# Two results of a doubling level in one PSUM bank, moved by one ScalarE copy

## The chip, the cores and the metric

One Trainium2 chip, of which the kernel uses one core. The metric is device time in microseconds (us), lower is better. The core has TensorE (PE in the rows; its weight loads are shown apart as PEld), VectorE (DVE), ScalarE (ACT), GpSimd (POOL) and SyncE (SP), each with its own in-order queue; they meet by semaphores.

## The reference

The computation has three parts: a delta-rule attention over 4 x 8 heads of 768 tokens with 48 channels, then a mixture of 8 experts with Sinkhorn routing, then a gated feed-forward. The change lies in the first:

```
k_n = k / (np.linalg.norm(k, axis=-1, keepdims=True) + 1e-06)
state = np.zeros((B, H, D, D), dtype=np.float32)
for t in range(S):
    kt, vt, bt = (k_n[:, :, t], v[:, :, t], beta[:, :, t, None])
    y[:, :, t] = np.einsum('bhd,bhde->bhe', q[:, :, t], state)
    v_old = np.einsum('bhde,bhd->bhe', state, kt)
    state = state + bt[:, :, :, None] * np.einsum('bhd,bhe->bhde', kt, vt - v_old)
...
logits = x @ w_gate      # routing, 8 Sinkhorn rounds, out += P[:, e] * (relu(x @ w1[e]) @ w2[e])
...
h = x @ w_in             # g = h * sigmoid(1.702 h), result g @ w_out
```

## The kernel before

The attention takes 4 heads at a time (8 groups) and cuts the 768 tokens into 6 chunks of 128. In a chunk the recurrence is a unit triangular system of 128 x 128 for each head. The kernel builds the inverse of that matrix by doubling: from blocks of 2 rows at level 1 to blocks of 128 after level 6. It keeps the inverse, x, and its transpose, xt, both in fp16, since TensorE wants the stationary operand transposed. A level is four steps:

1. level_y on TensorE (L298): the off-diagonal part of the matrix, a_r, times x, into a PSUM bank (the first product of a level);
2. level on VectorE (L569): that result times a mask, into yp in SBUF;
3. level_x (L309) and level_xt (L317) on TensorE: xt with yp gives the new blocks of x, yp with xt the new blocks of xt. L309 is the second product and L317 the transpose product. Level 6 has no level_x;
4. on ScalarE a copy of each into x (L460) and xt (L465), fp32 in the bank, fp16 in SBUF.

Two chunks, a pair, go through the levels together, as stream 0 and stream 1. Each step of a stream is four matmuls of 128x64, one for each head, so a row "x8" is the step of both streams. Each stream has two banks (2 + 2a + n % 2, b_lev at L175), in which level n's results alternate; of a bank only the first half, 256 fp32 words, is used.

There are 24 pairs (8 groups of 3). The program is written as one body for each pair, in which each engine does three things at three distances: the serial chain (ser) of pair p, the levels (dbl) of pair p + 1 and the preparation (pre) of pair p + 2. The order of the instructions in a body is written out by hand, on each engine by itself (TensorE L409 to L440, ScalarE L500 to L513, VectorE L640 to L661); nothing is reordered afterwards. Fifteen bodies out of the middle are five rounds of a loop on the device, the rest are written out. The chain of a chunk, on TensorE, is key_state (L332), solve (L344), product with lp (L355), correct (L365), outputs (L377 to L386). Ahead of product, correct and outputs stand 10, 10 and 4 filler matmuls on the identity (L324). grams (L279) and first_x (L287) belong to the preparation. In a body the first chunk's chain lies beside levels 1 to 3, and the second's beside levels 4 to 6.

Waits that matter here: the next level's L298 waits for the x copy of its stream (act_x), L309 for yp and for the level before's xt copy (act_xt), L355 for the copy of z0 (L469) on ScalarE, L365 for VectorE's residual (L594).

After the attention the dense part runs (L863 on), on TensorE nearly without gaps.

## Time and profile before

| | |
|---|---|
| median of 3 runs | 2610.67 us (2607.55 to 2611.66) |
| span of the profiled execution | 2601.5 us |
| between that span and the median of the runs | 9.2 us |
| TensorE matmul / weight load busy | 2491.3 us (96%) / 2238.2 us (86%) |
| VectorE, ScalarE, GpSimd busy | 1054.2 us (41%), 584.0 us (22%), 648.5 us (25%) |
| TensorE idle before L309, of it for VectorE's yp | 20.6 us, 11.4 us |
| TensorE idle before L298 (all at the loop's returns) | 11.6 us |

The profiled execution gives its span; its own time is not listed apart from those of the runs, so the span and the 9.2 us to the median are what a sum is made against. Matmuls overlap one another, so the start of a row to the start of the next says how long a group held the queue; the row's own length includes what the last matmul took to drain. A slice of the page is 65 us; the attention is the first eight. The granted clock (PEclk) is a share of 2.4 GHz.

### The profile page before, as it was taken

How to read it: one execution, taken by the hardware profiler on the slowest of the kernel's cores; microseconds unless marked ns; L12 is line 12 of the kernel's file. 1: busy time of each engine (PE TensorE's matmuls, PEld its weight loads, DVE VectorE, ACT ScalarE, POOL GpSimd, SP SyncE). 2: the span in 40 equal slices, each digit the busy share in tenths (PEclk: the TensorE clock that was granted, in tenths of full speed). 3: DMA queues.
4: the chain of work that ended last, by engine and by line, in shares of the span. 5: the costliest groups of instructions: out<-in, count | busy, mean ns of one | idle time of the engine just before them, and what ended most of it. 6: DMA issues, size and time to landing. Idle time of an engine off the chain costs nothing.

```text
span 2601.5 us, 42564 instructions
## 1 busy us (share of the span) xinstructions
PE 2491.3 (96%) x17329; PEld 2238.2 (86%) x17329; DVE 1054.2 (41%) x2147; ACT 584.0 (22%) x1326; POOL 648.5 (25%) x545
## 2 busy tenths in 40 slices
PE   6988889869999999999999999999999999999999
PEld 5877778738998998998998998998999999999998
DVE  5877778554333333333333333333333333223222
ACT  4444444321111111111111111111111112222222
POOL 5555555240100101101101001001001001444532
PEclk9999989979999999999999999999999999999999
DMA  2111111010000000000000000000000000000001
GB/s 76 49 45 45 45 45 55 22 43 7 25 1 24 25 1 26 13 12 25 13 13 25 13 13 25 13 13 25 13 13 25 1 25 1 25 13 13 13 13 61
DMA packets 54612, 61.72 MB, mean 24 GB/s; under 512 B 2336, under 2 KB 46624, under 8 KB 54432
## 3 DMA queue, kind: packets, MB, share of 16 engines
q1 hardware_dynamic: 54432, 58.97, 7.3%
q8 instruction: 156, 2.56, 0.4%
q14 instruction: 24, 0.20, 0.0%
HBM read 54.24 MB, written 4.72 MB: 23 GB/s over the span
## 4 chain that ended last, share of the span: by engine, by line
PE 78%; DVE 2%; issue 0%; ACT 0%
PE bank L955 38%; PE bank L928 38%; PE bank L874 1%; PE bank L907 0%; DVE x_hl L1085 0%; DVE rowsum L1165 0%; PE bank L973 0%; DVE route L1169 0%; DVE route L1181 0%; PE bank L863 0%; DVE gated L1080 0%; DVE h_hl L1103 0%; DVE gate_hl L1071 0%; ACT x_hl L994 0%; PE bank L882 0%
## 5 line engine op out<-in xcount | busy, mean ns | idle before, releaser
L928 PE MATMUL bank<-x_hl,w_hl 128*128 128x512 f32 x4320 | 1022.8, 394 | 2.9 <-issue 2.9
L955 PE MATMUL bank<-w_hl,h_hl 128*128 128x384 f32 x5760 | 1019.5, 335 | 0.0
L955 PEld LDWEIGHTS bank<-w_hl,h_hl 128*128 128x128 f32 x5760 | 1003.4, 188 | 10.0
L928 PEld LDWEIGHTS bank<-x_hl,w_hl 128*128 128x128 f32 x4320 | 811.5, 188 | 178.3 <-issue 4.5
L1014 ACT ACTIVATE h_hl<-bank 128x512 fp32r<-128x512 f32 x384 | 229.7, 598 | 1379.7 <-PE bank L928 1379.7
L1103 DVE SCALAR_TENSOR_TENSOR h_hl<-bank,h_hl 128x512 fp32r<-128x512 f32 x384 | 265.7, 692 | 584.7 <-ACT h_hl L1014 584.5
L808 POOL TENSOR_TENSOR w_hl<-w_raw,ones 128x1536 fp32r<-128x1536 f32 x40 | 109.9, 2748 | 1378.9 <-PE bank L928 1054.7
L1127 DVE SCALAR_TENSOR_TENSOR x_tok<-bank,route,x_tok 128x384 f32<-128x384 f32 x384 | 237.3, 618 | 499.2 <-PE bank L955 499.2
L849 POOL TENSOR_TENSOR h_hl<-gated,h_hl 128x512 fp32r<-128x512 f32 x96 | 123.4, 1291 | 318.8 <-ACT h_hl L1024 318.8
L814 POOL TENSOR_TENSOR w_hl<-w_raw,w_hl 128x1536 fp32r<-128x1536 f32 x40 | 140.7, 3518 | 2.7
L1116 DVE TENSOR_TENSOR gated<-bank,sig 128x512 f32<-128x512 f32 x96 | 66.4, 692 | 166.0 <-ACT sig L1033 117.6
L460 ACT CAST x<-bank 128x256 f16<-128x256 f32 x240 | 81.2, 375 | 182.3 <-PE bank L309 181.4
L1033 ACT ACTIVATE sig<-bank 128x512 f32<-128x512 f32 x96 | 57.4, 598 | 281.7 <-PE bank L928 281.7
L569 DVE TENSOR_TENSOR yp<-bank,mask 128x256 f16<-128x256 f32 x288 | 108.4, 418 | 26.2 <-PE bank L298 26.1
L709 POOL TENSOR_TENSOR a_r<-lp,mask 128x256 f16<-128x256 f32 x96 | 70.0, 729 | 175.9 <-DVE lp L558 175.9
L465 ACT CAST xt<-bank 128x256 f16<-128x256 f32 x288 | 94.8, 388 | 35.2 <-PE bank L317 33.2
L324 PE MATMUL bank<-ident 128*128 128x128 f16 x1152 | 92.6, 226 | 0.0
L558 DVE SCALAR_TENSOR_TENSOR lp<-bank,bg,mask 128x256 f32<-128x256 f32 x192 | 83.1, 476 | 11.7 <-PE bank L279 11.0
L309 PEld LDWEIGHTS bank<-yp,xt 128*128 128x128 f16 x960 | 46.7, 104 | 44.9 <-issue 27.0
L309 PE MATMUL bank<-yp,xt 128*128 128x64 f16 x960 | 58.0, 196 | 20.6 <-DVE yp L569 11.4
L298 PE MATMUL bank<-x,a_r 128*128 128x64 f16 x1152 | 64.1, 197 | 11.6 <-issue 10.6
L1139 DVE TENSOR_TENSOR x_tok<-x_tok,bank 128x384 f32<-128x384 f32 x72 | 39.9, 554 | 85.9 <-PE bank L955 85.9
(99 smaller groups left out, 1512.5 us busy)
## 6 DMA issues: line engine op xcount, KB each, us to landing
w_raw<-in_moe_w SPq DMA_DIRECT2D x32, 768.0 KB, 4.4
kq_t<-in_kq_rows SPq DMA_DIRECT2D x48, 256.0 KB, 3.3
kv<-in_kv_cols SPq DMA_DIRECT2D x24, 384.0 KB, 3.7
out<-x_tok SPq DMA_DIRECT2D x6, 768.0 KB, 3.5
w_raw<-in_moe_w_in SPq DMA_DIRECT2D x4, 768.0 KB, 4.3
w_raw<-in_moe_w_out SPq DMA_DIRECT2D x4, 768.0 KB, 4.5
mask<-in_masks SPq DMA_DIRECT2D x1, 576.0 KB, 4.6
beta_t<-in_beta_cols SPq DMA_DIRECT2D x1, 96.0 KB, 2.9
```

What stands on the lines that cost most here:

```text
L309: m = pe.matmul(b_lev(a, lev, lev)[:, u, :, :], xt[:, c, u, :], blocks(yp[:, a, lev - 1, :, :], lev, 0)[:, u, :, :], start=True, stop=True)
L324: pe.matmul(bank[:, b, 3 * P:4 * P], ident16[:, :], ident16[:, :], start=True, stop=True)
L465: act.copy(blocks(xt[:, c, :, :], lev, 1), b_lev(a, lev + 1, lev)).then_inc(act_xt[a], 1)
L569: dve.tensor_tensor(blocks(yp[:, a, lev - 1, :, :], lev, 0), b_lev(a, lev + 1, lev), keep.to_broadcast([P, GH, P >> (lev + 1), 1 << lev]), ...
L808: pool.tensor_tensor(dst[:, 0, :, :], raw[:, :, :], ones[:, 0:1].unsqueeze(2).to_broadcast([P, k, f]), ALU.mult).then_inc(pool_whi, 1)
L814: pool.tensor_tensor(dst[:, 1, :, :], raw[:, :, :], dst[:, 0, :, :].bitcast(F32), ALU.subtract).then_inc(pool_w, 1)
L849: pool.tensor_tensor(h_hl[:, s % 2, 1, f, :], gated[:, n % 2, :], h_hl[:, s % 2, 0, f, :].bitcast(F32), ALU.subtract).then_inc(pool_lo, 1)
L928: m = pe.matmul(bank[:, f, :], w1_hl[par][:, a, kc, f * P:(f + 1) * P], x_hl[:, c, kc, b * TB:(b + 1) * TB], start=n + kc == 0, stop=n == ...
L955: m = pe.matmul(bank[:, 4 + t, 0:DM], h_hl[:, b % 2, a, f, t * P:(t + 1) * P], w2_hl[par][:, c, f, :], start=n + f == 0, stop=n == len(PAR ...
L1014: act.activation(h_hl[:, b % 2, 0, f, :], bank[:, f, :], ACT.Relu).then_inc(act_h, 1)
L1103: dve.scalar_tensor_tensor(out=h_hl[:, b % 2, 1, f, :], in0=bank[:, f, :], scalar=0.0, in1=h_hl[:, b % 2, 0, f, :].bitcast(F32), op0=ALU.m ...
L1127: dve.scalar_tensor_tensor(out=dst, in0=bank[:, 4 + t, 0:DM], scalar=route[:, b * TT + t, col], in1=dst, op0=ALU.mult, op1=ALU.add).then_i ...
```

## The change

x and xt become the two planes of one buffer xx, for each chunk plane 0 for x and plane 1 for xt. The new x blocks of a level lie in plane 0 at even positions and the new xt blocks in plane 1 at odd ones, so one access pattern with a step between planes (grown) reaches both. In PSUM each stream now has one bank instead of two: its first half takes level_y's result and then, once VectorE has read that, level_x's; its second half takes level_xt's. ScalarE moves both halves with one copy on levels 1 to 5; level 6 has xt alone, as before. The four semaphore pairs pe_x, act_x, pe_xt, act_xt become two, pe_xx_lev (raised behind level_xt) and act_xx_lev (raised by the copy). level_y of a level waits for act_xx_lev, on level 1 also for the last copy of the pair before, since the bank is now the same. level_x waits for VectorE alone. Banks 4 and 5 are no longer used by the levels.

```diff
@@ -117,10 +117,8 @@
             sem, ("pe_g", "dve_lp", "pool_at", "pool_xt", "pe_x1", "act_x1"))
         pe_y = [sem(f"pe_y_stream{a}") for a in range(2)]
         dve_y = [sem(f"dve_y_stream{a}") for a in range(2)]
-        pe_x = [sem(f"pe_x_stream{a}") for a in range(2)]
-        act_x = [sem(f"act_x_stream{a}") for a in range(2)]
-        pe_xt = [sem(f"pe_xt_stream{a}") for a in range(2)]
-        act_xt = [sem(f"act_xt_stream{a}") for a in range(2)]
+        pe_xx_lev = [sem(f"pe_xx_lev_stream{a}") for a in range(2)]
+        act_xx_lev = [sem(f"act_xx_lev_stream{a}") for a in range(2)]
         pe_ks, dve_r, dve_rl, pe_z0, act_z0 = map(sem, ("pe_ks", "dve_r", "dve_rl", "pe_z0", "act_z0"))
         pe_az, dve_res, dve_resl, pe_xr, dve_z = map(sem, ("pe_az", "dve_res", "dve_resl", "pe_xr", "dve_z"))
         pe_kz, pe_out, dve_state, act_yo = map(sem, ("pe_kz", "pe_out", "dve_state", "act_yo"))
@@ -156,8 +154,8 @@
 
             lp = sb("lp", [P, NCH, GH, 2 * P], ctx=at)
             a_r = sb("a_r", [P, NCH, GH, P], F16, ctx=at)
-            xt = sb("xt", [P, NCH, GH, P], F16, ctx=at)
-            x = sb("x", [P, NCH, GH, P], F16, ctx=at)
+            xx = sb("xx", [P, NCH, 2, GH, P], F16, ctx=at)
+            x, xt = xx[:, :, 0, :, :], xx[:, :, 1, :, :]
 
 
             yp = sb("yp", [P, 2, NLEV - 1, GH, P], F16, ctx=at)
@@ -172,10 +170,21 @@
 
             BT, BS, BO = 0, 6, 7
 
-            def b_lev(a, n, lev):
-
-                return bank[:, 2 + 2 * a + n % 2, 0:GH * P // 2].rearrange(
+            def b_lev(a, w, lev):
+
+                return bank[:, 2 + a, w * GH * P // 2:(w + 1) * GH * P // 2].rearrange(
                     "p (u m r) -> p u m r", u=GH, r=1 << lev)
+
+            def grown(c, lev):
+
+                r = 1 << lev
+                first = xx[:, c, 0, 0, 0:1]
+                return bass.AP(first.tensor, first.offset,
+                               [first.ap[0], [GH * P + r, 2], [2 * r, GH * P // (2 * r)], [1, r]])
+
+            def b_grown(a, lev):
+
+                return bank[:, 2 + a, :].rearrange("p (w m r) -> p w m r", w=2, r=1 << lev)
 
             def blocks(t, lev, odd):
 
@@ -291,32 +300,31 @@
                         a = c % 2
                         if lev == 1:
                             pe.wait_ge(act_x1, j + 1)
+                            wait(pe, act_xx_lev[a], (NLEV - 1) * p)
                         else:
 
-                            pe.wait_ge(act_x[a], (NLEV - 2) * p + lev - 1)
+                            pe.wait_ge(act_xx_lev[a], (NLEV - 1) * p + lev - 1)
                         for u in range(GH):
-                            m = pe.matmul(b_lev(a, lev + 1, lev)[:, u, :, :], a_r[:, c, u, :],
+                            m = pe.matmul(b_lev(a, 0, lev)[:, u, :, :], a_r[:, c, u, :],
                                           blocks(x[:, c, :, :], lev, 0)[:, u, :, :], start=True, stop=True)
                         m.then_inc(pe_y[a], 1)
 
                     def level_x(g, c, j, p, lev):
                         a = c % 2
 
-                        wait(pe, act_xt[a], (NLEV - 1) * p + lev - 1)
                         pe.wait_ge(dve_y[a], (NLEV - 1) * p + lev)
                         if lev < NLEV - 1:
                             for u in range(GH):
-                                m = pe.matmul(b_lev(a, lev, lev)[:, u, :, :], xt[:, c, u, :],
-                                              blocks(yp[:, a, lev - 1, :, :], lev, 0)[:, u, :, :],
-                                              start=True, stop=True)
-                            m.then_inc(pe_x[a], 1)
+                                pe.matmul(b_lev(a, 0, lev)[:, u, :, :], xt[:, c, u, :],
+                                          blocks(yp[:, a, lev - 1, :, :], lev, 0)[:, u, :, :],
+                                          start=True, stop=True)
 
                     def level_xt(g, c, j, p, lev):
                         a = c % 2
                         for u in range(GH):
-                            m = pe.matmul(b_lev(a, lev + 1, lev)[:, u, :, :], yp[:, a, lev - 1, u, :],
+                            m = pe.matmul(b_lev(a, 1, lev)[:, u, :, :], yp[:, a, lev - 1, u, :],
                                           blocks(xt[:, c, :, :], lev, 1)[:, u, :, :], start=True, stop=True)
-                        m.then_inc(pe_xt[a], 1)
+                        m.then_inc(pe_xx_lev[a], 1)
 
                     def keep_busy(b, n):
 
@@ -338,7 +346,7 @@
 
                         wait(pe, act_yo, j)
                         pe.wait_ge(dve_rl, j + 1)
-                        pe.wait_ge(act_xt[c % 2], (NLEV - 1) * (p + 1))
+                        pe.wait_ge(act_xx_lev[c % 2], (NLEV - 1) * (p + 1))
                         for u in range(GH):
                             for n in range(2):
                                 m = pe.matmul(b_ser(BO)[:, u, :], xt[:, c, u, :], rhs_hl[:, n, u, :],
@@ -454,15 +462,13 @@
                         act.wait_ge(pe_x1, j + 1)
                         act.copy(x[:, c, :, :], b_x1()).then_inc(act_x1, 1)
 
-                    def level_x(g, c, p, lev):
+                    def level(g, c, p, lev):
                         a = c % 2
-                        act.wait_ge(pe_x[a], (NLEV - 2) * p + lev)
-                        act.copy(blocks(x[:, c, :, :], lev, 0), b_lev(a, lev, lev)).then_inc(act_x[a], 1)
-
-                    def level_xt(g, c, p, lev):
-                        a = c % 2
-                        act.wait_ge(pe_xt[a], (NLEV - 1) * p + lev)
-                        act.copy(blocks(xt[:, c, :, :], lev, 1), b_lev(a, lev + 1, lev)).then_inc(act_xt[a], 1)
+                        act.wait_ge(pe_xx_lev[a], (NLEV - 1) * p + lev)
+                        if lev < NLEV - 1:
+                            act.copy(grown(c, lev), b_grown(a, lev)).then_inc(act_xx_lev[a], 1)
+                        else:
+                            act.copy(blocks(xt[:, c, :, :], lev, 1), b_lev(a, 1, lev)).then_inc(act_xx_lev[a], 1)
 
                     def solved(g, c, j):
                         act.wait_ge(pe_z0, j + 1)
@@ -481,11 +487,8 @@
                         def levels(lev):
                             if dbl is not None:
                                 g, c, p = dbl
-                                if lev < NLEV - 1:
-                                    level_x(g, c, p, lev)
-                                    level_x(g, c + 1, p, lev)
-                                level_xt(g, c, p, lev)
-                                level_xt(g, c + 1, p, lev)
+                                level(g, c, p, lev)
+                                level(g, c + 1, p, lev)
 
                         def prep(a, what):
                             if pre is not None:
@@ -566,7 +569,7 @@
                         a = c % 2
                         dve.wait_ge(pe_y[a], (NLEV - 1) * p + lev)
                         keep = blocks(mask[:, LEVEL + lev:LEVEL + lev + 1, :], lev, 0)
-                        dve.tensor_tensor(blocks(yp[:, a, lev - 1, :, :], lev, 0), b_lev(a, lev + 1, lev),
+                        dve.tensor_tensor(blocks(yp[:, a, lev - 1, :, :], lev, 0), b_lev(a, 0, lev),
                                           keep.to_broadcast([P, GH, P >> (lev + 1), 1 << lev]),
                                           ALU.mult).then_inc(dve_y[a], 1)
 
```

On ScalarE the levels of a body change as follows, levels 4 and 5 of one body, with the second chunk's z0 copy and the roots of a later pair between them. Before (xt and x are the two buffers, pe_x and pe_xt TensorE's two products):

```order
L460 CAST x<-bank 128x16x16 [waits pe_x_stream0]
L460 CAST x<-bank 128x16x16 [waits pe_x_stream1]
L465 CAST xt<-bank 128x16x16 [waits pe_xt_stream0]
L465 CAST xt<-bank 128x16x16 [waits pe_xt_stream1]
L469 COPY z<-bank 128x192 [waits pe_z0]
L451 ACTIVATE root<-ss 128x8 [waits dve_ss]
L460 CAST x<-bank 128x8x32 [waits pe_x_stream0]
L460 CAST x<-bank 128x8x32 [waits pe_x_stream1]
L465 CAST xt<-bank 128x8x32 [waits pe_xt_stream0]
L465 CAST xt<-bank 128x8x32 [waits pe_xt_stream1]
```

and after, at the same place (xx is the shared buffer):

```order
L469 CAST xx<-bank 128x2x16x16 [waits pe_xx_lev_stream0]
L469 CAST xx<-bank 128x2x16x16 [waits pe_xx_lev_stream1]
L475 COPY z<-bank 128x192 [waits pe_z0]
L459 ACTIVATE root<-ss 128x8 [waits dve_ss]
L469 CAST xx<-bank 128x2x8x32 [waits pe_xx_lev_stream0]
L469 CAST xx<-bank 128x2x8x32 [waits pe_xx_lev_stream1]
```

Four copies of 256 columns have become two of twice 256, and the wait is on the later of the two products. No other instruction of ScalarE changes its place.

TensorE's matmuls keep their order; what they wait for changes. Before, from level 4's first product to level 5's (grams, then level 4's second and transpose products, then solve):

```order
L298 MATMUL bank<-x,a_r 128x64 [waits act_x_stream0]
L298 MATMUL bank<-x,a_r 128x64 x3
L298 MATMUL bank<-x,a_r 128x64 [waits act_x_stream1]
L298 MATMUL bank<-x,a_r 128x64 x3
L279 MATMUL bank<-kq_t 128x256 [waits act_x1,ld_kq5]
L279 MATMUL bank<-kq_t 128x256 x3
L309 MATMUL bank<-yp,xt 128x64 [waits dve_y_stream0,act_xt_stream0]
L309 MATMUL bank<-yp,xt 128x64 x3
L309 MATMUL bank<-yp,xt 128x64 [waits dve_y_stream1,act_xt_stream1]
L309 MATMUL bank<-yp,xt 128x64 x3
L317 MATMUL bank<-xt,yp 128x64 x8
```

and after, at the same place:

```order
L308 MATMUL bank<-xx,a_r 128x64 [waits act_xx_lev_stream0]
L308 MATMUL bank<-xx,a_r 128x64 x3
L308 MATMUL bank<-xx,a_r 128x64 [waits act_xx_lev_stream1]
L308 MATMUL bank<-xx,a_r 128x64 x3
L288 MATMUL bank<-kq_t 128x256 [waits act_x1,ld_kq5]
L288 MATMUL bank<-kq_t 128x256 x3
L318 MATMUL bank<-yp,xx 128x64 [waits dve_y_stream0]
L318 MATMUL bank<-yp,xx 128x64 x3
L318 MATMUL bank<-yp,xx 128x64 [waits dve_y_stream1]
L318 MATMUL bank<-yp,xx 128x64 x3
L325 MATMUL bank<-xx,yp 128x64 x8
```

The first product's wait has moved from the x copy to the copy of both, and the second product's wait for ScalarE is gone.

## Rows read from the trace of the kernel before

**Rows 1.** page, busy tenths in 40 slices, and the chain that ended last by engine.

```profile
PE   6988889869999999999999999999999999999999
...
PE 78%; DVE 2%; issue 0%; ACT 0%
```

**Rows 2.** busy time by stretches: PE, PEld, DVE, ACT, POOL (x instructions), PEclk, DMA share, GB/s.

```profile
98.80:108.60 9.80, 8.06 (x146) 7.41 (x146) 7.96 (x23) 4.61 (x15) 5.34 (x8) 1.00 0.23 70
276.10:285.90 9.80, 5.51 (x91) 4.67 (x90) 6.59 (x19) 2.66 (x8) 4.90 (x8) 0.95 0.23 70
285.90:295.80 9.90, 9.38 (x108) 9.38 (x108) 4.14 (x12) 3.21 (x10) 4.80 (x6) 0.53 0.01 3
305.60:315.50 9.90, 8.90 (x147) 7.96 (x147) 8.44 (x26) 4.18 (x13) 5.43 (x9) 1.00 0.21 68
```

**Rows 3.** timeline, levels 3 and 4: start us, us, engine, line, what, [idle before].

```profile
316.30 0.40 PE L317 MATMUL bank<-xt,yp 128*128 128x64 f16 x8
...
316.53 0.40 PE L298 MATMUL bank<-x,a_r 128*128 128x64 f16 x8
...
316.85 0.73 PEld L279 LDWEIGHTS bank<-kq_t 64*128 64x128 f32 x8
316.86 1.13 PE L279 MATMUL bank<-kq_t 64*128 64x256 f32 x8
...
317.50 0.75 DVE L569 TENSOR_TENSOR yp<-bank,mask 128x256 f16<-128x256 f32 x2
...
317.97 0.70 PE L309 MATMUL bank<-yp,xt 128*128 128x64 f16 x8
...
318.50 0.40 PE L317 MATMUL bank<-xt,yp 128*128 128x64 f16 x8
...
318.74 0.36 PE L344 MATMUL bank<-rhs_hl,xt 128*128 128x48 bf16 x8
...
318.94 0.48 PE L298 MATMUL bank<-x,a_r 128*128 128x64 f16 x8
...
319.26 0.72 PE L324 MATMUL bank<-ident 128*128 128x128 f16 x10
319.50 0.35 ACT L469 COPY z<-bank 128x192 f32<-128x192 f32 x1
...
319.98 0.97 PEld L355 LDWEIGHTS bank<-z,lp 128*128 128x128 f32 x8 [0.17 <-POOL a_r L709]
```

**Rows 4.** timeline, level 5.

```profile
320.90 0.40 PE L309 MATMUL bank<-yp,xt 128*128 128x64 f16 x8
...
321.14 0.40 PE L317 MATMUL bank<-xt,yp 128*128 128x64 f16 x8
321.22 0.65 ACT L460 CAST x<-bank 128x256 f16<-128x256 f32 x2 [1.27 <-PE bank L309]
...
322.63 0.37 PE L365 MATMUL bank<-res_hl,xt 128*128 128x48 bf16 x8 [0.54 <-DVE res_hl L594]
...
322.84 0.39 PE L298 MATMUL bank<-x,a_r 128*128 128x64 f16 x8
```

**Rows 5.** timeline, level 6 and level 1 of the next pair.

```profile
325.29 0.40 PE L317 MATMUL bank<-xt,yp 128*128 128x64 f16 x8
...
326.03 0.40 PE L298 MATMUL bank<-x,a_r 128*128 128x64 f16 x8
...
327.82 0.70 PE L309 MATMUL bank<-yp,xt 128*128 128x64 f16 x8 [0.33 <-DVE yp L569]
```

**Rows 6.** groups by line, whole run: busy us, mean ns | idle before.

```profile
L569 DVE TENSOR_TENSOR yp<-bank,mask 128x256 f16<-128x256 f32 x288 | 108.4, 418 | 26.2 <-PE bank L298 26.1
L465 ACT CAST xt<-bank 128x256 f16<-128x256 f32 x288 | 94.8, 388 | 35.2 <-PE bank L317 33.2
...
L460 ACT CAST x<-bank 128x256 f16<-128x256 f32 x240 | 81.2, 375 | 182.3 <-PE bank L309 181.4
...
L455 ACT COPY x<-bank 128x512 f16<-128x512 f16 x48 | 28.1, 585 | 55.4 <-PE bank L287 55.4
```

## The prediction

> **What bounds the kernel now.** I read the page first, for where the end is set. The chain that ended last is TensorE for 78% of the span, and it lies in the dense part, where TensorE is at nine tenths or more in every slice [rows 1]. The change touches nothing there. It touches the attention part, the first eight of the forty slices, which ends at about 520 us. The dense part waits for all of it, so what attention gains or loses moves the end one for one. In attention TensorE is at eight to nine tenths, its in-order queue being the longest of the five. The second view is the busy time by stretches: in an ordinary stretch of 9.9 us TensorE is busy for 8.90, VectorE for 8.44 and ScalarE for 4.18 [rows 2]. ScalarE, whose work the change cuts, has more than half its time free. So fewer ScalarE instructions are worth something only where TensorE waits for one. The third view, the timeline, shows how little it waits now.
>
> Call S the start of the transpose product of a level (L317). The rows give, for level 3, S = 316.30: the next level's first product (L298) starts at S + 0.23, the grams (L279) at S + 0.56, level 4's second product (L309) at S + 1.67 and its transpose product at S + 2.20 [rows 3]. For level 4, S = 318.50: solve (L344) at S + 0.24, L298 at S + 0.44, the ten filler products (L324) at S + 0.76, and the product with lp (L355) at S + 1.48, after a wait of 0.17 [rows 3]. For level 5, S = 321.14: the correction (L365) at S + 1.49, L298 at S + 1.70 [rows 4]. For level 6, S = 325.29: L298 at S + 0.74, and L309 a full 2.53 us behind S [rows 5]. Levels 1 and 2 of the next pair repeat levels 4 and 5, since the serial chain stands in the same places.
>
> **What goes away.** As the order of ScalarE's instructions shows, each level from 1 to 5 has four ScalarE copies of 128x256 now, and two of 128x512 after. The whole run has 240 x copies of 375 ns and 288 xt copies of 388 ns [rows 6]; 240 of each become 240 larger ones, 48 stay. That relieves an engine with time to spare. Also gone is level_x's wait for the xt copy of the level before, and the trace has next to nothing waiting there: L309 waits for VectorE. I put both at nothing.
>
> **What is added.** Now x is copied while TensorE still runs the transpose product, and the next L298 follows that copy alone. After the change one copy needs both products, so it cannot start before the transpose product has written, and L298 needs its end. A wait appears on TensorE's in-order queue, with everything of the serial chain and of the next pair queued behind it.
>
> How long it is: a copy starts 0.32 us after the product that feeds its stream has begun (L309 at 320.90, copy at 321.22 [rows 4]). The trace has no fp32-to-fp16 copy of 128x512, so its price is bounded. From below: no more than a 128x256 one, 0.375. From above: two such copies behind one another, 0.65 us for the pair [rows 4]. The nearest row is the ScalarE copy of 128x512 fp16 out of a bank, 585 ns [rows 6], and I take 0.59. For the second stream, two 256 copies take 0.65 together, so the second starts 0.27 behind the first; the larger one adds 0.59 - 0.38 = 0.21, giving 0.48. Stream 0 is then copied at S + 0.91 and stream 1 at S + 1.39. With about 0.06 for the signal (estimate: L309 at 317.97 starts 0.05 after the first of the VectorE pair at 317.50 [rows 3] has run its 0.418 [rows 6]), L298 runs its first half at S + 0.97, its second at S + 1.45, and TensorE is free of it at about S + 1.56.
>
> The Trainium skill bears on the same size. "ScalarE: Activation LUTs", section on what ACT_TABLE_LOAD costs, gives 186 ns plus 0.833 ns an element for an activation with immediates, and an overlap of about 93 ns between neighbours. By it the copy would be 613 ns, the pitch 520, and the second end 0.06 us later than mine, which over the 72 places below is 4 us more. The two rows lie a little under that rule (375 against 399 for 256, 585 against 613 for 512), so the rows are used.
>
> Level by level:
> - Levels 4 and 1: L298 used to be done at S + 0.76. Now S + 1.56, then the ten fillers (0.55 in the queue), and L355 at S + 2.11 where it was S + 1.48. The ScalarE copy of z0 ends near S + 1.39 + 0.35 = S + 1.74, before that, so the old wait of 0.17 is swallowed. Cost 0.63 each, 1.26 a pair.
> - Level 3: L298's second half at S + 1.45, grams 0.22 behind it at S + 1.67 and over at S + 2.41 (their weight loads take 0.73 [rows 3], and I round up to the 0.74). VectorE has both yp by then: it is free at 317.50, S + 1.20, starts the second 0.32 after that half's product, at S + 1.77, and ends it at S + 2.19. Level 4's L309 starts at S + 2.41, but it no longer stalls between its halves, so its transpose product starts 0.23 behind (as on level 5 [rows 4]) at S + 2.64, where it was S + 2.20. Cost 0.44 a pair.
> - Levels 5 and 2: the copies end at S + 1.39, the correction starts at S + 1.49 anyway for VectorE's sake, L298 at S + 1.70. Cover: the serial chain's own wait, with 0.25 to spare. Nothing.
> - Level 6 into level 1 of the next pair: one copy per stream as before, but L298 now writes into the same bank and so waits for it: second half near S + 0.32 + 0.65 + 0.06 = S + 1.03 against S + 0.85. L309 stands 2.53 us behind S for VectorE's sake, and that hides 0.18. Without key_state ahead of it (one body in three) L298 slips by up to 0.54, and L309 waits there too. Nothing.
>
> Sum: 1.26 + 0.44 = 1.70 us a pair. 240 x copies are 24 pairs of 5 levels and 2 streams, so 24 pairs: 41 us. The profiled execution has a span of 2601.5; with 41 it is 2642. The median of the runs is 2610.67, 9.2 above the span, and that part doesn't move: 2652.
>
> The ends. With copies at their lower bound (0.375, pitch 0.27) the second ends at S + 0.97: levels 4 and 1 cost 0.21 each, level 3 nothing, in all 0.42 x 24 = 10 us: 2621. With 0.65 for a copy and as much for the pitch, the second ends at S + 1.62, everything 0.23 later than in my sum: 1.70 + 3 x 0.23 = 2.4, 57 us: 2668.
>
> **Rivals.**
> Rival A, the clock falls. TensorE's granted clock is 1.00, which is 2.4 GHz, in nearly all stretches, and goes towards 0.5 (1.2 GHz) after the stall at the loop's return, where TensorE was busy for 5.51 of 9.8 us [rows 2]. The change adds two idle pieces at three places a pair. In the low stretch 108 matmuls run in 9.9 us against 147 at full clock [rows 2], so 9.9 us there lose 2.6. If the clock were low for half of the 510 us of attention, that is 26 stretches by 2.6, 67 us on top: 2719. Against it: by my sum a stretch of 9.9 becomes about 10.75 with the same 8.90 busy, 83%, and the row at 98.80 has 8.06 of 9.80, 82%, at clock 1.00; no new gap is near the 2.6 us that stand ahead of the fall. Chance 11%.
> The Trainium skill argues for this rival: "TensorE: Matmul & The Clock Gate", section on a second failure mode, tells of a kernel that cycled through PSUM banks and idled briefly between groups of matmuls often enough for the clock to swing. By that rule the time would be rival A's; the row at 98.80 is against it at this size of gap.
>
> Rival B, cover that I don't see. If the copies cost what their lower bound says and the fillers behind L298 absorb the rest of the wait, nothing is left: 2611, up to the 2621 above. For it: the fillers are there only to keep TensorE running, and the product behind them waited 0.17. Against it: they are instructions in the queue and run however late they are. Chance 8%.
>
> Rival C, faster: ScalarE is drained sooner. z0's copy is queued behind the level's copies, and L355 waits 0.17 for it. If two large copies end before the four small ones did (319.50 is when z0's copy starts, S + 1.00), L355 starts earlier, by 0.17 at most, in 48 places: 8 us, 2603. It decides only if the second merged copy ends before S + 1.00, so copy and pitch together under 0.68, and if L298's added wait is then also under the 0.17. Two copies of twice the size at 585 ns don't do that. Chance 4%.
>
> **Chances.** Forecast 77%, A 11%, B 8%, C 4%. The forecast's own range is 2621 to 2668; I stretch it upwards to take in the nearer half of the clock's cases and a pitch larger than assumed: 2625 to 2685. A measurement here can tell about 0.2%, 5 us. Slower by more than that: the forecast and A, 88%. Within: most of B, 7%. Faster: C and a little more, 5%.
>
> **What the profile after would show.** ScalarE copies of 128x512 fp16 from fp32, 240 of them, near 590 ns; TensorE waiting for ScalarE ahead of both halves of the next first product after levels 1, 3 and 4, in all some 1 us each time, and not after 2 and 5; L355's wait gone; ScalarE busy for less, attention ending near 560 us; the granted clock as before outside the loop's returns. It is wrong if the copies are much off 590, if level 3 costs as much as level 4 (then VectorE's stall was no cover), if levels 2 and 5 wait too, or if low clock shows in stretches where it was 1.00.

## The result and the profile after

The changed kernel takes 2639.91 us (median of 4 runs, 2630.43 to 2644.35) against 2611.07 before (4 runs, 2607.55 to 2611.66): ratio 1.0119, interval 1.0101 to 1.0136. It is slower by about 29 us (31 by the ratio); the forecast was 2652, 41 slower.

The loss is in attention. The dense part's first instruction starts at 546.91 us in the profile after and at 520.26 before, 26.7 of the 27.1 by which the spans differ (2628.6 and 2601.5). The page shows the same chain behind it [rows 1]:

```profile
PE   6888888877999999999999999999999999999999
...
PE 77%; DVE 2%; issue 0%; ACT 0%
```

The added wait is there and so is the copy's size. Groups by line of the changed kernel (line numbers are its own: L469 is the merged copy, L308 the first product, L597 the low part of the residual, which is the fp32 residual less its bf16 rounding):

```profile
L469 ACT CAST xx<-bank 128x512 f16<-128x512 f32 x240 | 128.8, 589 | 249.1 <-PE bank L325 249.1
...
L308 PE MATMUL bank<-xx,a_r 128*128 128x64 f16 x1152 | 80.0, 196 | 59.9 <-ACT xx L469 45.1 <-issue 11.4 <-ACT xx L471 1.8
...
L597 DVE TENSOR_TENSOR res_hl<-res,res_hl 128x192 bf16<-128x192 f32 x48 | 17.2, 357 | 1.6
```

240 merged copies at 589 ns stand for 480 at 375 to 388 [rows 6]. L308 now idles TensorE for 45.1 us behind L469, where its namesake L298 had no wait for ScalarE worth a row. The waits of TensorE for it in 50 to 540 us, in total, times, longest:

```profile
PE bank L308 <- ACT xx L469: 41.8, 135, 0.6
```

Levels 3 and 4 in the timeline, to be laid beside [rows 3]. S is 331.54:

```profile
331.54 0.40 PE L325 MATMUL bank<-xx,yp 128*128 128x64 f16 x8
...
331.85 1.07 ACT L469 CAST xx<-bank 128x512 f16<-128x512 f32 x2 [2.26 <-PE bank L325]
...
332.49 0.29 PE L308 MATMUL bank<-xx,a_r 128*128 128x64 f16 x4 [0.56 <-ACT xx L469]
...
332.82 0.91 DVE L572 TENSOR_TENSOR yp<-bank,mask 128x256 f16<-128x256 f32 x2
...
332.98 0.29 PE L308 MATMUL bank<-xx,a_r 128*128 128x64 f16 x4 [0.20 <-ACT xx L469]
...
333.20 1.14 PE L288 MATMUL bank<-kq_t 64*128 64x256 f32 x8
334.26 0.29 PEld L318 LDWEIGHTS bank<-yp,xx 128*128 128x128 f16 x8 [0.33 <-issue]
334.27 0.41 PE L318 MATMUL bank<-yp,xx 128*128 128x64 f16 x8
...
334.51 0.40 PE L325 MATMUL bank<-xx,yp 128*128 128x64 f16 x8
```

The first product runs in two halves at S + 0.95 and S + 1.44, each behind its half of the copy, which took 1.07 for the pair. grams follows at S + 1.66. VectorE has both yp by 332.82 + 0.91 = S + 2.19. The second product starts at S + 2.73, after 0.33 in which no engine is named. Then level 4, S = 334.51:

```profile
334.83 1.07 ACT L469 CAST xx<-bank 128x512 f16<-128x512 f32 x2 [1.68 <-PE bank L325]
...
335.47 0.29 PE L308 MATMUL bank<-xx,a_r 128*128 128x64 f16 x4 [0.36 <-ACT xx L469]
...
335.96 0.29 PE L308 MATMUL bank<-xx,a_r 128*128 128x64 f16 x4 [0.20 <-ACT xx L469]
...
336.59 0.97 PEld L363 LDWEIGHTS bank<-z,lp 128*128 128x128 f32 x8
...
337.52 0.40 PE L318 MATMUL bank<-yp,xx 128*128 128x64 f16 x8
...
337.76 0.40 PE L325 MATMUL bank<-xx,yp 128*128 128x64 f16 x8
```

The weight loads of L363 (the product with lp) start at S + 2.08 and without the old wait. Last the residual of level 5, S = 337.76:

```profile
337.57 0.73 POOL L712 TENSOR_TENSOR a_r<-lp,mask 128x256 f16<-128x256 f32 x1 [0.56 <-DVE lp L561]
...
337.73 0.35 DVE L594 TENSOR_TENSOR res_hl<-rhs,bank 128x192 bf16<-128x192 f32 x1 [0.23 <-PE bank L363]
...
338.38 0.36 DVE L597 TENSOR_TENSOR res_hl<-res,res_hl 128x192 bf16<-128x192 f32 x1
338.39 0.88 POOL L715 TENSOR_TENSOR xx<-a_r,mask 128x256 f16<-128x256 f16 x1
...
338.79 0.37 PE L373 MATMUL bank<-res_hl,xx 128*128 128x48 bf16 x8
```

The correction (L373) starts at S + 1.03. Before it was S + 1.49 [rows 4]. The low part of the residual takes 0.36, and GpSimd's L715, which starts at the same moment, takes 0.88 instead of its usual 0.67. In the kernel before the pair looked the other way round. Its timeline at the same place:

```profile
320.87 0.73 POOL L709 TENSOR_TENSOR a_r<-lp,mask 128x256 f16<-128x256 f32 x1 [0.20 <-DVE lp L558]
...
321.11 0.36 DVE L591 TENSOR_TENSOR res_hl<-rhs,bank 128x192 bf16<-128x192 f32 x1 [0.31 <-PE bank L355]
...
321.69 0.67 POOL L712 TENSOR_TENSOR xt<-a_r,mask 128x256 f16<-128x256 f16 x1
...
321.76 0.81 DVE L594 TENSOR_TENSOR res_hl<-res,res_hl 128x192 bf16<-128x192 f32 x1
...
322.63 0.37 PE L365 MATMUL bank<-res_hl,xt 128*128 128x48 bf16 x8 [0.54 <-DVE res_hl L594]
```

GpSimd starts 0.07 earlier there, and VectorE's instruction takes 0.81. In the changed kernel all 48 low parts take 357 to 359 ns. In the kernel before 34 of the 48 take 478 to 878 (median of the 48: 812), and 14 take 357 or 358. The 14 lie in bodies at the two ends of attention: in four no GpSimd instruction runs beside them, in one it is all but over, and in nine it starts between 3 ns ahead of VectorE's and 17 behind, and takes 0.87 to 0.89 itself. So the kernel before has both outcomes in one run, and some nanoseconds decide: 6 ahead were enough for GpSimd. In the changed kernel its start lies between 4 ahead and 11 behind.

What moved the two starts can be read from the rows, from level 4's transpose product (318.50 before, 334.51 after). GpSimd's a_r (L709 before, L712 after), which waits for VectorE's lp and stands right ahead of GpSimd's xt, went from S + 2.37 to S + 3.06, by 0.69. VectorE's residual (L591 before, L594 after), which follows the product with lp, went from S + 2.61 to S + 3.22, by 0.61. GpSimd lost 0.08 against VectorE, and it had been 0.07 ahead.

From one transpose product to the next, medians over the bodies at full clock, from the starts in the timelines (us):

| from level to level | 3 to 4 | 4 to 5, 1 to 2 (each) | 5 to 6 | 6 to 1 | 2 to 3 | a pair |
|---|---|---|---|---|---|---|
| before | 2.21 | 2.63 | 4.16 | 3.07 | 4.89 | 19.59 |
| changed | 2.98 | 3.25 | 3.80 | 3.07 | 4.53 | 20.88 |
| forecast of the difference | +0.44 | +0.63 | 0 | 0 | 0 | +1.70 |
| measured | +0.77 | +0.62 | -0.36 | 0.00 | -0.36 | +1.29 |

One body in three is 0.45 shorter from 5 to 6 and from 2 to 3, in both kernels, so the differences hold for it too. 1.29 by 24 pairs is 31 us. Some of it comes back at the loop's returns: the first correction of the run is 2.7 us late, the 36th 16.9 and the 48th 26.6, but at two of the returns the lag falls, from 16.9 to 15.1 and from 17.4 to 14.1. In these two profiled executions the low clock after a return is shorter in the changed kernel. Busy time by stretches, with one that holds a return and an ordinary one [rows 2]:

```profile
167.80:177.60 9.80, 6.76 (x92) 5.57 (x92) 5.24 (x16) 1.97 (x6) 2.77 (x6) 0.83 0.24 71
...
305.60:315.50 9.90, 8.51 (x145) 7.40 (x144) 6.98 (x20) 4.36 (x10) 4.41 (x7) 1.00 0.10 28
```

Behind the four returns together the clock is at its low level for 14 us, where it was for 38 before. At 2.6 us lost in 9.9 [rows 2] the 24 us of difference are worth some 6, an estimate. Over the spans the mean clock is 0.986 after and 0.982 before.

### The profile page after: what moved, and what is told of

The parts are those of the page before. It is cut to its first block, busy times and chain, and to the rows that moved or that the text cites. A ratio compares the mean times of both kernels' runs of the same rounds, so it can differ in the third digit from the quotient of the medians.

```text
span 2628.6 us, 42033 instructions
## 1 busy us (share of the span) xinstructions
PE 2503.0 (95%) x17329; PEld 2236.6 (85%) x17329; DVE 1051.0 (40%) x2147; ACT 563.2 (21%) x1086; POOL 651.9 (25%) x545
## 4 chain that ended last, share of the span: by engine, by line
PE 77%; DVE 2%; issue 0%; ACT 0%
PE bank L958 38%; PE bank L931 38%; PE bank L877 1%; PE bank L910 0%; DVE x_hl L1088 0%; PE bank L976 0%; DVE route L1172 0%; DVE route L1184 0%; PE bank L866 0%; DVE gated L1083 0%; DVE h_hl L1106 0%; DVE gate_hl L1074 0%; ACT x_hl L997 0%; DVE rowsum L1168 0%; PE bank L885 0%
## 5 line engine op out<-in xcount | busy, mean ns | idle before, releaser
L469 ACT CAST xx<-bank 128x512 f16<-128x512 f32 x240 | 128.8, 589 | 249.1 <-PE bank L325 249.1
L308 PE MATMUL bank<-xx,a_r 128*128 128x64 f16 x1152 | 80.0, 196 | 59.9 <-ACT xx L469 45.1
L572 DVE TENSOR_TENSOR yp<-bank,mask 128x256 f16<-128x256 f32 x288 | 115.3, 420 | 42.3 <-PE bank L308 37.5
L308 PEld LDWEIGHTS bank<-xx,a_r 128*128 128x128 f16 x1152 | 51.2, 98 | 82.2 <-ACT xx L469 62.5
L712 POOL TENSOR_TENSOR a_r<-lp,mask 128x256 f16<-128x256 f32 x96 | 69.8, 727 | 204.0 <-DVE lp L561 204.0
L715 POOL TENSOR_TENSOR xx<-a_r,mask 128x256 f16<-128x256 f16 x96 | 74.0, 771 | 7.5
L288 PE MATMUL bank<-kq_t 64*128 64x256 f32 x384 | 62.9, 452 | 9.4 <-DMA kq_t<-in_kq_rows 8.5
```

The costliest lines, as they stand in the source:

```text
L308: m = pe.matmul(b_lev(a, 0, lev)[:, u, :, :], a_r[:, c, u, :], blocks(x[:, c, :, :], lev, 0)[:, u, :, :], start=True, stop=True)
L469: act.copy(grown(c, lev), b_grown(a, lev)).then_inc(act_xx_lev[a], 1)
L572: dve.tensor_tensor(blocks(yp[:, a, lev - 1, :, :], lev, 0), b_lev(a, 0, lev), keep.to_broadcast([P, GH, P >> (lev + 1), 1 << lev]), ALU.m ...
```

## The experiments

A ratio is to the kernel before on the same chip. Steps from level to level are medians as in the table above.

**e1_split: the shared buffer, the copies apart.** The changed kernel with xt's result in a bank of its own, two copies a stream, and the first product waiting for the x copy alone.

```diff
-                return bank[:, 2 + a, w * GH * P // 2:(w + 1) * GH * P // 2].rearrange(
+                return bank[:, 2 + a + 2 * w, 0:GH * P // 2].rearrange(
...
-                            pe.wait_ge(act_xx_lev[a], (NLEV - 1) * p + lev - 1)
+                            pe.wait_ge(act_x[a], (NLEV - 2) * p + lev - 1)
...
-                            act.copy(grown(c, lev), b_grown(a, lev)).then_inc(act_xx_lev[a], 1)
+                        act.copy(blocks(x[:, c, :, :], lev, 0), b_lev(a, 0, lev)).then_inc(act_x[a], 1)
+                        act.copy(blocks(xt[:, c, :, :], lev, 1), b_lev(a, 1, lev)).then_inc(act_xt[a], 1)
```

> The changed kernel with the shared buffer xx kept, level_y and level_x of a stream still in one bank, but level_xt's result in a bank of its own and two copies on ScalarE again, so that the next level's first product waits for the x copy alone. Theory (the wait for the merged copy is the whole cost, less what an accident of the VectorE and GpSimd timing gives back): everything returns, 2611 within 4 us, the low part of the residual back at 0.81 us. Rival (the layout of the shared buffer, or one bank for the first and second product, costs something of itself): stays above 2616.

2610.88 us, ratio 1.0004 (0.9995 to 1.0013). Every row of the table above is back to before, within 0.01, and the low part has a median of 807 ns again. The buffer's layout and the one bank for first and second product cost nothing.

**e2_wait_only: the wait alone, nothing merged.**

```diff
                             pe.wait_ge(act_x[a], (NLEV - 2) * p + lev - 1)
+                            pe.wait_ge(act_xt[a], (NLEV - 1) * p + lev - 1)
```

> The kernel before with one line more: the next level's first product also waits for the xt copy of its stream. Four small copies, four banks, no merging. Theory: the wait is what costs, and the merged copy's size comes on top of it. With small copies the second stream's xt copy ends near S + 1.13 (level 4) in place of S + 1.39, so levels 1 and 4 cost about 0.37 each and level 3 about 0.4; if the residual's low part stays at 0.81 that is 1.1 us a pair, 2638; if it falls to 0.36 on levels 2 and 5 it is some 0.4 a pair, 2620. Rival (a wait on small copies is free since they run beside the transpose product, and all the cost is the copy's size): 2611.

2637.33 us, ratio 1.0108 (1.0093 to 1.0123). Level 3 to 4 takes 2.62 (+0.41), 4 to 5 3.21 (+0.58) and 1 to 2 3.06 (+0.42, expected +0.37 for each), and 5 to 6 and 2 to 3 are 0.36 shorter, the low part at 358 ns in 44 of 48. 6 to 1 takes 3.16 (+0.09). That is +0.79 a pair, 19 us, and the run lost 26 to 29. The rest isn't the wait for ScalarE. TensorE's waits show it under "issue":

```profile
PE bank L299 <- ACT xt L466: 30.2, 66, 0.6
PE bank L299 <- issue: 25.7, 8, 3.9
```

25.7 us in 8 pauses, against 11.4 in 4 in the changed kernel. All eight lie at the loop's four returns: one ahead of the first L299 of a body, as in every kernel here, and one of 3.3 to 3.9 us behind that single matmul, ahead of the other seven. What makes the second is open; it belongs to e2 alone, and the steps above don't contain it. The rival, a free wait, is out: the wait on small copies costs three fifths of what the merged copy costs (+0.79 against +1.29 a pair). The other 0.50 comes with the merged copy, which is larger and starts only behind the transpose product, 0.35 of it at level 3.

**e3_before_res: one SBUF input fewer.** The kernel before with the fp32 residual in PSUM.

```diff
-                        dve.tensor_tensor(res[:, :, :], rhs[:, :, :], b_ser(BS), ALU.subtract)
+                        dve.tensor_tensor(b_res(), rhs[:, :, :], b_ser(BS), ALU.subtract)
...
-                        dve.tensor_tensor(res_hl[:, 1, :, :], res[:, :, :], res_hl[:, 0, :, :], ALU.subtract
+                        dve.tensor_tensor(res_hl[:, 1, :, :], b_res(), res_hl[:, 0, :, :], ALU.subtract
```

b_res() is columns 192 to 383 of bank BS, which no matmul writes between the product and the correction.

> The kernel before with the fp32 residual written into unused columns of its own PSUM bank instead of SBUF, so that the VectorE instruction that forms the low part has one SBUF input instead of two. Theory (that instruction at 0.81 us was waiting for a GpSimd instruction that began 0.07 us before it; in the changed kernel it began just ahead and took 0.36): it takes about 0.36 in all 48 chunks, the correction starts up to 0.46 earlier, and the kernel ends 16 to 22 us earlier, 2589 to 2595. Rival (the 0.81 is that instruction's own time on this path, and in the changed kernel it is shorter since ScalarE is less busy): unchanged, 2611.

2590.34 us, ratio 0.9929 (0.9916 to 0.9943), inside the forecast and faster than both kernels. Its timeline at level 5:

```profile
322.34 0.67 POOL L714 TENSOR_TENSOR xt<-a_r,mask 128x256 f16<-128x256 f16 x1
...
322.41 0.36 DVE L596 TENSOR_TENSOR res_hl<-bank,res_hl 128x192 bf16<-128x192 f32 x1
...
322.83 0.37 PE L367 MATMUL bank<-res_hl,xt 128*128 128x48 bf16 x8
```

GpSimd again starts 0.07 ahead, as before, and VectorE takes 0.36 all the same, since only one of its inputs is in SBUF. In the run all 48 lie between 356 and 358 ns. Levels 5 to 6 and 2 to 3 are down to 3.71 and 4.44, by 0.45 each.

**e4_after_res: the same edit to the changed kernel.**

> The changed kernel with the same edit to the residual. Theory (in the changed kernel VectorE already wins the race for the read port, in the profiled run in all 48 chunks, so there is nothing left to gain): 2640, within 5 us; the spread of its runs (2630 to 2644) would shrink if they come from races lost now and then. Rival (ScalarE's load set the 0.36): 2640 as well, but then the kernel before with this edit stays at 2611. Second rival (a PSUM write costs VectorE more than an SBUF write): slower than 2645.

2639.15 us, ratio 1.0106 (1.0083 to 1.0129), runs from 2627.1 to 2644.07. No gain, as expected, since the race was already won. The spread did not shrink, so lost races don't make it. The profiled runs point at the clock: 2642.47 us at a mean of 0.978 here, 2630.43 at 0.986 in the changed kernel, with the steps of the levels alike but for 6 to 1, which is 0.2 shorter here. With the clock at 0.5 where it is low, that is 116 us of low clock against 74 (twice the missing share of the span); at 2.6 us lost in 9.9 [rows 2] the 42 us are worth 11 of the 12 between the runs. That is an estimate and not varied by an edit.

e3 and e4 also give the price of the change with the race out of both kernels: 2590.34 against 2639.15, 49 us. By levels it is +0.77 (3 to 4), +0.61 each (4 to 5, 1 to 2), +0.08 and +0.09 (5 to 6, 2 to 3) and -0.08 (6 to 1), 2.08 a pair. So levels 5 and 2 do pay a little. Once the correction starts at S + 1.03, the second half of the next first product waits for the copy: it follows the first half by 0.20 there in the changed kernel, and by 0.11 in the kernel before and e3.

**e5_nudge and e9_nudge_wide: GpSimd starts later.** The kernel before, with a memset of an unused tile on GpSimd between a_r and xt of a chunk's second half; 64 columns in e5, 384 in e9.

```diff
+                        if m == 1:
+                            pool.memset(spare[:, :], 0.0)
                         pool.wait_ge(pool_at, 3 * j + m + 1)
```

> The kernel before with nothing changed on VectorE, TensorE or ScalarE; GpSimd alone gets a small extra instruction (a memset of 64 columns of an unused tile) between a_r and xt of the second half of a chunk, so that its xt instruction begins some 0.1 us or more later. Theory (an exclusive claim on the SBUF read port, won by whoever starts first): VectorE's low part of the residual now starts first, takes 0.36 in place of 0.81, GpSimd waits instead, and the kernel is faster although it does more: 2588 to 2597. Rival (the low part is slow for another reason): 2611 or more, the low part at 0.81.

2606.97 us, ratio 0.9988 (0.9979 to 0.9997): the forecast missed, and the low part stayed at 819 ns. The edit did not do what it was to do:

```profile
333.61 0.15 POOL L713 MEMSET spare<- 128x64 f32 x1
333.75 0.67 POOL L715 TENSOR_TENSOR xt<-a_r,mask 128x256 f16<-128x256 f16 x1
...
333.81 0.83 DVE L595 TENSOR_TENSOR res_hl<-res,res_hl 128x192 bf16<-128x192 f32 x1
```

The memset filled the pause that stood behind a_r anyway, and xt still starts 0.06 ahead of the low part. So this run tells nothing between the theories, and the wider one followed.

> As e5_nudge, whose 64-column memset lay in the pause between two GpSimd instructions and moved the start of xt by nothing against VectorE's low part (323.88 against 323.95); now the memset has 384 columns and should last some 0.4 us, so that xt begins 0.1 to 0.4 us behind the low part. Theory (the read port goes to whoever starts first): the low part at 0.36 in nearly all 48 chunks, levels 2 and 5 shorter by 0.36 each, the kernel 16 to 20 us faster than before although GpSimd does more, 2589 to 2597. Rival (the port is not it): the low part stays at 0.81 and the time at 2610.

2593.97 us, ratio 0.9956 (0.9941 to 0.9970), inside the forecast, low part at 357 or 358 ns in 43 of 48:

```profile
337.82 0.42 POOL L713 MEMSET spare<- 128x384 f32 x1
...
338.04 0.36 DVE L595 TENSOR_TENSOR res_hl<-res,res_hl 128x192 bf16<-128x192 f32 x1
338.20 0.73 POOL L715 TENSOR_TENSOR xt<-a_r,mask 128x256 f16<-128x256 f16 x1
```

Now xt starts 0.16 behind the low part. 5 to 6 takes 3.80 and 2 to 3 takes 4.52, as in the changed kernel. GpSimd does more, and the kernel is 14 us faster. So the order of two starts is worth that much, with the instructions of VectorE, ScalarE and TensorE untouched.

**e10_after_dnudge: VectorE starts later, in the changed kernel.**

```diff
+                        dve.memset(spare[:, 0:16], 0.0)
                         dve.wait_ge(dve_res, j + 1)
```

> The changed kernel with the opposite nudge: VectorE gets a memset of 16 columns of an unused tile between the fp32 residual and its low part, so that the low part begins after GpSimd's xt instruction and not with it. Theory: the low part falls back to about 0.8 us, levels 2 and 5 are some 0.36 to 0.5 longer, and the change costs what my sum said and more: 48 x 0.4 = 19 us above the changed kernel, 2655 to 2665. Rival (the 0.36 of the changed kernel comes from a less busy ScalarE or the free banks): only the memset's own tenth of a microsecond, about 2644.

2634.07 us, ratio 1.0122 (1.0100 to 1.0145): missed. As in e5 the 0.07 us memset fitted into a pause (the low part ahead of or level with GpSimd's instruction, 327.66 and 327.67, and at 357 ns in all 48). So this run doesn't show the changed kernel with the race lost; e7 below does, by a third route.

**e6_after_grams: grams into the gap.** The changed kernel with two lines swapped.

```diff
-                        levels(4, level_y)
                         prep(1, grams)
+                        levels(4, level_y)
```

> The changed kernel with grams put ahead of level 4's first product on TensorE, into the wait for the merged copy. What is tested is the third of a microsecond between the end of grams and the matmuls behind them, which my sum lacked. Theory (it belongs to grams: the next weight load waits until their last matmul has drained): the gap of about 0.33 moves with grams and now stands ahead of level 4's first product, whose first half starts near S + 1.29; from level 3's transpose product to level 4's some 2.35 in place of 2.97; 15 us faster than the changed kernel, about 2625. Rival (it belongs to the second product, a signal from VectorE that comes late): first product at S + 0.97 still, no gap behind grams, the second product as late after its yp as before; about 2630.

2628.24 us, ratio 1.0069 (1.0055 to 1.0083). Level 3 to 4 takes 2.66 (2.98 in the changed kernel, 2.35 expected). The first product after grams:

```profile
332.61 1.13 PE L288 MATMUL bank<-kq_t 64*128 64x256 f32 x8
...
333.67 0.29 PEld L308 LDWEIGHTS bank<-xx,a_r 128*128 128x128 f16 x8 [0.33 <-issue]
```

L308 follows grams by 1.06, the same distance at which the second product followed grams in the changed kernel (333.20 to 334.27), and this time the idle piece stands ahead of L308. So it belongs to grams and was hidden before by L309's wait for VectorE. Whether the drain of the last matmul makes it is not shown. Level 3 to 4 stays above the expected 2.35 since the first product comes at S + 1.39, not 1.29, and the second product, which then waits for VectorE's yp again, at S + 2.20.

**e7_after_fill: the filler into the gap as well.** As e6, and the ten filler matmuls of the product ahead of the next first product.

```diff
                         chain(0, solve, True)
+                        chain(0, fill)
                         levels(2, level_y)
...
                         chain(1, solve, True)
+                        chain(1, fill)
                         levels(5, level_y)
```

> As the run before, and in addition the ten filler matmuls of the product stand ahead of the first product of levels 2 and 5 instead of behind it, so that they run in the wait for the merged copy. Theory (the whole cost of the change is TensorE standing still at three places a pair while its filler work waits behind): levels 1 and 4 fall from 3.25 to about 2.7 us (2.63 in the kernel before), in all about 2600 if the residual's low part stays at 0.36, and 2618 if its race is lost again. Rival (the merged copy costs by itself, through ScalarE or the shared bank): stays above 2620 with the low part at 0.36.

2614.80 us, ratio 1.0024 (1.0015 to 1.0033). 25 of the 29 us are back, 15 short of the forecast. Levels 1 and 4 take 2.90, not 2.7. The forecast's 2600 assumed the low part at 0.36; it is at 0.46 (L600, median 462 ns). The timeline from level 4's transpose product (334.99), with level 5's at 337.89:

```profile
334.99 0.40 PE L325 MATMUL bank<-xx,yp 128*128 128x64 f16 x8
...
335.43 0.72 PE L332 MATMUL bank<-ident 128*128 128x128 f16 x10
...
335.98 0.28 PE L308 MATMUL bank<-xx,a_r 128*128 128x64 f16 x4
...
336.43 0.29 PE L308 MATMUL bank<-xx,a_r 128*128 128x64 f16 x4 [0.17 <-ACT xx L472]
...
336.73 1.09 PE L364 MATMUL bank<-z,lp 128*128 128x48 f32 x8
337.10 0.87 DVE L564 SCALAR_TENSOR_TENSOR lp<-bank,bg,mask 128x256 f32<-128x256 f32 x2
...
337.89 0.40 PE L325 MATMUL bank<-xx,yp 128*128 128x64 f16 x8
338.05 0.73 POOL L715 TENSOR_TENSOR a_r<-lp,mask 128x256 f16<-128x256 f32 x1 [0.83 <-DVE lp L564]
...
338.53 0.46 DVE L600 TENSOR_TENSOR res_hl<-res,res_hl 128x192 bf16<-128x192 f32 x1
338.86 0.67 POOL L718 TENSOR_TENSOR xx<-a_r,mask 128x256 f16<-128x256 f16 x1
...
339.05 0.37 PE L374 MATMUL bank<-res_hl,xx 128*128 128x48 bf16 x8 [0.20 <-DVE res_hl L600]
...
339.58 0.40 PE L296 MATMUL bank<-ident,xx 128*128 128x128 f16 x4
```

The fillers hide the wait of the first half, but the second half still runs at S + 1.44 and the product with lp can only stand behind it, at S + 1.74. At level 5 something else is late. GpSimd's a_r, which follows VectorE's lp pair, starts at S + 0.16, against S - 0.19 in the changed kernel (337.57). It now begins 0.48 ahead of the low part, which takes 0.46, so the correction comes 1.16 behind the transpose product and not 1.03. GpSimd's xt ends at 338.86 + 0.67, and first_x (L296), which reads it, starts 0.05 behind that. 5 to 6 takes 3.93. e8 tells which of the two sets it.

**e8_after_fill_res: both.**

> The run before with the fp32 residual in PSUM, so that no race decides. Theory: level for level like the kernel before with the residual in PSUM (2590), plus 0.1 to 0.2 us a pair for what the gaps don't cover: 2590 to 2600. Rival (a merged copy is worth something once its wait is covered, ScalarE being drained sooner): below 2588.

2613.75 us, ratio 1.0021 (1.0010 to 1.0032): missed by 14 us, and not told apart from e7. The low part is at 357 ns and the correction at S + 1.06, but 5 to 6 stays at 3.93. So first_x behind GpSimd's xt sets that step, and not the correction: in the median it starts 0.06 behind the end of xt, in e7 and in e8. GpSimd is late because the lp pair is, and that pair stands behind a yp that waits for the second half of the copy.

e8 is 23 us slower than e3, which has four small copies. The rival, a gain from a shorter ScalarE queue, is not seen; but the wait is not covered in full here either (0.17 ahead of each second half, with the product with lp behind it), so e8 doesn't exclude a small one. In e3 there is little left to gain between 50 and 515 us: TensorE's weight loads wait 4.4 us in all, 26 times up to 0.2, ahead of the product with lp, where the z0 copy can be the cause, and 1.4 us once ahead of solve.

## Why the prediction was right, and where its terms were off

The mechanism of the wait stood: x's copy used to run beside the transpose product, the merged one cannot, and the three places without cover pay. e1 takes the wait away and the loss is gone; e2 adds only the wait and most of the loss is there.

- The copy. Forecast 0.59 and a second end at S + 1.39; measured 589 ns and, in level 4, 334.83 + 1.07 = S + 1.39.
- Levels 4 and 1, 0.63 each: measured 0.62.
- Level 3, 0.44: measured 0.77. The term mis-sized is grams, which I ended at S + 2.41 by its weight loads. The step from grams to anything behind it has 0.33 more. In the kernel before, VectorE's wait lay over it, so no row named it there. e6 moved it with grams. The prediction gave "level 3 costs as much as level 4" as a sign of being wrong, and it came true (0.77 against 0.62), though not for the reason it named: VectorE had its yp at S + 2.19, as forecast.
- Levels 5 and 2, "nothing", since "the correction starts at S + 1.49 anyway for VectorE's sake": measured -0.36 each, 17 us over 24 pairs. This is the step that failed. I took VectorE's wait for a fixed length of work. It held 0.45 of waiting for GpSimd, decided by 0.07 us, and the change's own delay of the lp instructions, behind which GpSimd is queued, shifted GpSimd by 0.08 more than VectorE. e3 and e9 show the 0.45 and how it goes away; that the shift came about in this way in the changed kernel is worked out from its timeline, and no edit varied it alone (in e7, which shifts GpSimd too, the low part is long again). The -0.36 is -0.45 for this and +0.09 for the copy (e3 and e4), whose cover of 0.25 went with the early correction.
- Level 6 into 1, nothing: measured 0.00 to 0.01.
- The clock, rival A: not seen. In the profiled execution it was low for less time than before, and that returns some 6 of the 31 us (estimate above).
- Rival B needed copies at their lower bound of 0.375, and they took 0.589. Fillers ahead of the wait recover most of it (e7); behind the wait, where they stood, they cover none of it. Rival C needed copy and pitch under 0.68 together, and they took 1.07.
- Attention ending "near 560 us": 546.9. The waits ahead of the first product, "some 1 us each time": 0.76 at level 3 and 0.56 at level 4.

1.26 + 0.77 - 0.72 = 1.31 a pair for the sum with the two terms put right, 31 us, against 29 measured. The forecast of 41 lies as near as it does by luck in part: an error of +0.33 a pair stands against one of -0.72. With the race out of both kernels the change costs 49 us. The 9.2 us that the prediction adds from the span to the median are mostly spread: in every other run here the execution is 1.8 us above its own span. As they are added to both sides, the difference stays.

The Trainium skill has the race. "SBUF — State Buffer", section on who interferes with whom, says that a VectorE instruction with two SBUF inputs contends with a GpSimd instruction that reads SBUF, by an exclusive lock that goes to whoever issues first, and that with one SBUF input it doesn't. The traces agree: 812 ns with two inputs and GpSimd 0.07 ahead, 357 with VectorE level or ahead while GpSimd's instruction grows from 0.67 to 0.88, 358 with one input and GpSimd ahead. They also bear out the lock by its size. In all 34 long cases of the kernel before, and in all 44 of e7, the low part lasts its own 0.357 plus what was left of GpSimd's instruction when it started, less 0.14: 0.01 behind the start of 0.67 it takes 0.88, 0.48 behind the start of 0.73 it takes 0.46. GpSimd's 0.88 is the same sum the other way, 0.67 + 0.357 - 0.14. The prediction did not weigh that rule, which would have split the 0.81 into work and waiting.

## What to carry to other kernels

Before two results share a copy, ask what runs between the first result and the second. Here it was the transpose product on TensorE, with the x copy beside it, and fewer instructions on an engine that is half idle bought a wait on the engine that is not. Where a wait can't be avoided, put independent work ahead of the waiting instruction (e7 got back 25 of 29 us); fillers behind it cover nothing. And when an instruction on the path has a duration of twice its sister's (812 against 357 ns for the same form, L594 and L586), look for who started just ahead of it before taking it as a cost: here that was worth 18 to 21 us (e3), two thirds of what the change cost. Compare two kernels with such a race taken out of both: 29 us here were 49 less 20.

## What the runs showed of the hardware

- VectorE's 128x192 fp32 subtraction with both inputs in SBUF takes 357 ns, or some 810 when a GpSimd instruction that reads SBUF began 0.07 us earlier. With GpSimd 0.16 later it is 358. Whoever starts second lasts as long as its own work and the rest of the other's, less 0.14 us; in the kernel before a lead of 6 ns was enough for GpSimd, and one of 3 ns was not.
- Such a VectorE instruction is recorded as busy and not as waiting: the rows name VectorE where TensorE waits, and GpSimd nowhere.
- A delay of less than the pause ahead of an instruction does nothing: memsets of 0.15 us on GpSimd and 0.07 on VectorE moved the next instruction's start by at most a hundredth against the other engine.
- After a group of 64-row fp32 matmuls of 128x256 (grams), the next 128-row fp16 matmul starts 1.06 to 1.07 us behind the group's start, though its weight loads take 0.73; 0.33 us is idle.
- A ScalarE copy with two planes of 256 columns from a bank into fp16 SBUF takes 589 ns, close to the 585 of a plain copy of 512 columns, and 1.07 us for two in a row.
- Three added pauses in each 21 us body, of 0.56 to 0.76 us and each in two parts with matmuls between, did not lower TensorE's granted clock away from the loop's returns (1.00 in the stretch at 305.60 above).
